# Unused buffers between the weights of a fused convolution and two-layer-pair kernel

## The reference, cut to what matters

```python
# x: (2, 4096, 192); weight: (8, 7); w_in: (192, 2048); w_out: (2048, 192), two sets of these
w = softmax(weight, axis=-1)                               # 8 heads, 7 taps
x_pad = concat([zeros(B, 6, D), x], axis=1)
x = sum over k of w[head, k] * x_pad[:, s + k, channels of head]   # causal convolution
# first pair of layers
h = x @ w_in
g = where(h >= 1, h, where(h <= -1, 0, (h + 1) ** 2 / 4))
x = g @ w_out
# second pair of layers
h = x @ moe2_w_in
g = h * sigmoid(1.702 * h)
out = g @ moe2_w_out                                       # (8192, 192)
```

## Time and profile before

| what | value |
|---|---|
| median of three runs | 1173.59 us (1173.38 to 1175.2) |
| the profiled execution | 1176.4 us, of which the span from first to last instruction is 1174.6 |
| mean granted TensorE clock | 0.999 of full speed |
| matmuls recorded | 9382 |
| moved by DMA | 31.27 MB |

### The profile page before, as it was taken

The page is one execution under the profiler, slowest core; times in us unless marked ns, Lnnn a source line. Parts: engine busy times, 40 slices in busy tenths (PEclk is TensorE's granted clock), DMA queues, the critical chain, the costliest instruction groups (busy, mean ns, idle before and its releaser), DMA issues.

```text
span 1174.6 us, 25920 instructions
## 1 busy us (share of the span) xinstructions
PE 1146.1 (98%) x9382; PEld 1011.3 (86%) x9382; DVE 844.6 (72%) x1206; ACT 799.3 (68%) x1510; POOL 432.3 (37%) x425
## 2 busy tenths in 40 slices
PE   7999999999999999999999999999999999999998
PEld 4767898998988889888888889889898888999987
DVE  6877768686776868768686786867768686676633
ACT  4866676767758677686766767677686766855554
POOL 5897626080440805327071350905317071000000
PEclk9999999999999999999999999999999999999999
DMA  6312101001010000101001010010101000000001
GB/s 193 97 37 75 35 1 48 1 10 40 1 48 1 15 35 2 47 1 48 2 8 41 1 49 1 12 37 1 49 1 48 1 7 9 2 15 2 14 2 28
DMA packets 63857, 31.27 MB, mean 27 GB/s; under 512 B 56084, under 2 KB 60562, under 8 KB 63760
## 3 DMA queue, kind: packets, MB, share of 16 engines
q1 hardware_dynamic: 63760, 29.80, 9.6%
HBM read 23.09 MB, written 6.29 MB: 25 GB/s over the span
## 4 chain that ended last, share of the span: by engine, by line
PE 73%; DVE 8%; ACT 8%; issue 5%; POOL 4%; SPq 1%; DMA 0%; DVEq 0%; ACTq 0%; POOLq 0%
PE acc_all L764 3%; PE acc_all L756 2%; PE acc_all L742 2%; PE acc_all L761 2%; PE acc_all L759 2%; PE acc_all L767 2%; DVE g_lo L1115 2%; PE h_all L697 2%; PE h_all L699 2%; PE h_all L694 2%; ACT clip L938 2%; PE h_all L701 2%; PE h_all L703 2%; PE acc_all L738 2%; PE acc_all L740 2%
## 5 line engine op out<-in xcount | busy, mean ns | idle before, releaser
L1115 DVE TENSOR_TENSOR g_lo<-gate,g_hi 128x512 fp32r<-128x512 f32 x232 | 205.1, 884 | 92.2 <-ACT g_hi L944 87.3
L1121 DVE TENSOR_TENSOR g_lo<-h_all,g_hi 128x512 fp32r<-128x512 f32 x256 | 175.7, 686 | 124.8 <-ACT h_all L955 122.5
L944 ACT ACTIVATE g_hi<-gate 128x512 fp32r<-128x512 f32 x232 | 146.5, 632 | 166.2 <-DVE gate L1109 131.4
L938 ACT ACTIVATE clip<-clip,half 128x512 f32<-128x512 f32 x256 | 184.9, 722 | 60.5 <-DVE clip L1100 58.0
L952 ACT ACTIVATE g_hi<-h_all 128x512 fp32r<-128x512 f32 x256 | 152.9, 597 | 94.6 <-PE h_all L705 66.7
L510 POOL TENSOR_TENSOR x_conv<-x_in,tap_w 128x384 f32<-128x384 f32 (+1 forms) x29 | 24.7, 872 | 515.9 <-ACT raw L990 513.4
L1100 DVE TENSOR_SCALAR clip<-h_all 128x512 f32<-128x512 f32 x256 | 174.9, 683 | 20.8 <-PE h_all L703 17.3
L517 POOL TENSOR_TENSOR x_conv<-x_conv,prod 128x384 f32<-128x384 f32 (+1 forms) x174 | 187.5, 1098 | 1.6
L1109 DVE TENSOR_TENSOR gate<-h_all,clip 128x512 f32<-128x512 f32 x232 | 160.5, 692 | 35.7 <-ACT clip L938 24.1
L510 POOL TENSOR_TENSOR prod<-x_in,tap_w 128x384 f32<-128x384 f32 (+1 forms) x174 | 176.4, 1038 | 4.2
L955 ACT ACTIVATE h_all<-h_all 128x512 f32<-128x512 f32 x256 | 151.6, 592 | 0.0
(11 more groups left out here) (281 smaller groups left out, 4763.2 us busy)
## 6 DMA issues: line engine op xcount, KB each, us to landing
x_in<-in_x SPq DMA_DIRECT2D x14, 960.0 KB, 4.7
out_y<-raw SPq DMA_DIRECT2D x360, 16.0 KB, 1.4
raw<-in_moe_w_out SPq DMA_DIRECT2D x6, 384.0 KB, 3.5
raw<-in_moe_w_in SPq DMA_DIRECT2D x4, 512.0 KB, 4.5
raw<-in_moe_w_in SPq DMA_DIRECT2D x8, 256.0 KB, 4.8
stage<-in_moe_w_out SPq DMA_DIRECT2D x2, 384.0 KB, 7.4
x_in<-in_x SPq DMA_DIRECT2D x1, 768.0 KB, 8.7
x_in<-in_x SPq DMA_DIRECT2D x2, 283.5 KB
```

Of the source, the lines that this page charges most:

```text
L938: nc.scalar.activation(c, c, ACT.Square, bias=half[:, :], scale=0.5).then_inc(square_ready, 1)
L944: nc.scalar.activation(g1_hi[step.s % G_RING][:, :], gate1_of(step)[:, :], ACT.Copy).then_inc(g1_hi_ready, 1)
L1115: nc.vector.tensor_tensor(g1_lo[k][:, :], gate1_of(step)[:, :], g1_hi[k][:, :].bitcast(FP32), ALU.subtract).then_inc(g1_lo_ready, 1)
L1121: nc.vector.tensor_tensor(g2_lo[k][:, :], bank2(step)[:, :], g2_hi[k][:, :].bitcast(FP32), ALU.subtract).then_inc(g2_lo_ready, 1)
```

## The change

Five buffers are added that no instruction reads or writes. `sb(name, [P, size // 4])` takes `size` bytes in each partition, so that all buffers after it begin that much later. Nothing else is changed. By the words of the change, the streamed operands begin at 0 of 512 bytes with it, in_hi and w_down too, in_lo at 32, rest_hi at 448 and rest_lo at 256.

```diff
+        def shift(name, size):
+            sb(name, [P, size // 4])
+
+        shift("to_in_hi", 384)
         in_hi = [sb(f"in_hi{m}", [P, FF], FP32R) for m in (1, 2)]
+        shift("to_in_lo", 32)
         in_lo = [sb(f"in_lo{m}", [P, FF], FP32R) for m in (1, 2)]
+        shift("to_rest_hi", 416)
         rest_hi = [sb(f"rest_hi{m}", [P, FF], FP32R) for m in (1, 2)]
+        shift("to_rest_lo", 320)
         rest_lo = [sb(f"rest_lo{m}", [P, FF], FP32R) for m in (1, 2)]
+        shift("to_w_down", 256)
         w_down = [sb(f"w_down{m}", [P, F_TILES, 2 * D], FP32R) for m in (1, 2)]
```

## The result

| | before | with the change |
|---|---|---|
| median | 1173.49 us (10 runs) | 1177.80 us (10 runs) |
| ratio | 1 | 1.0037, 95% interval 1.0027 to 1.0047 |
| profiled execution | 1176.4 us, span 1174.6 | 1177.45 us, span 1175.7 |
| shortest step (5th percentile of 231) | 4306 ns | 4333 ns |
| median step | 4333 ns | 4360 ns |

The kernel became 4.3 us slower (3.2 to 5.5 by the interval); faster was forecast. The profiled execution of before lay 2.9 us over its median, so the two spans show only 1.1 us of it. The steps are read from the starts of the first matmul of `end_up` (L694, now L703; all lines of PE are nine further down).

What follows compares the result with a forecast made beforehand. PE's matmul pace was taken to bound the kernel, with waits for g_lo in 28% of steps. From the profiled 1176.4 us, 6.0 came off, giving 1170.4, or 1167.5 against the runs' median; DVE, ACT and DMA at zero; range 1127 to 1183.

Steps and rivals of the forecast that it cites:

- the separation into absolute and relative movement: All operands leave 128 of 512 bytes; only in_lo, rest_hi and rest_lo move against the stream, 1256 of 4700 slots.
- C: Rival, up pairs: weight loads at 32, 448 and 256 meet the stream and one halts; 1181 us, at most 1186; chance 0.20.
- Price of a slot: Step pricing each PE matmul slot whose weights move against the stream: half of the 13.4 ns rest vanishes, -6.7 ns.
- the 13.4 ns over 512 columns: Part of each 227 ns PE matmul beyond 213.3 ns for its columns, 32 cycles; taken as changeable by addresses.
- the term of -8.4 us (6.0 arriving): PE's gain: 1256 slots at 6.7 ns, of which 0.72 reaches the kernel's time.
- B: Rival, every matmul: the 13.4 ns is a fixed price that knows no addresses, so nothing changes; 1173.6 us; chance 0.29.
- 1160 paired slots: Paired steps: in_lo twice, rest_hi twice, rest_lo once, 5 of 19 pairs over 232 steps; 96 single slots came on top.
- 0.72: Share of PE's gain taken to arrive, since 28% of the steps wait for g_lo at L742.
- Rival D: All 4700 slots: streams start at a 512-byte edge, so aligning removes the whole rest; 45 us, 1128.5 us; chance 0.13.

Runs made afterwards that it cites:

- e1: Kernel before plus one unused 384-byte buffer ahead of in_hi, so every weight and streamed operand begins at 0 of 512 bytes: ratio 1.0003.
- e2: The change without its first buffer: same distances between operands, all standing 384 bytes lower; ratio 1.0021 against the kernel before.
- e5: Kernel before with only rest_lo moved, 256 bytes from the place of the streamed operands: ratio 0.9994.
- m1: Separate kernel of matmuls alone, 40 per group, weights' and stream's starts varied in 32-byte steps: 226.7 ns at distances 0 and 256, up to 234.2 at others.
- m2: Separate kernel, PE alone, rings of ten weights, some moved, also narrower weights: ten matmuls 2266.7 ns with none moved, 2286.7 with one at 32.
- e8: Kernel before with only w_down moved, 32 bytes from the place of the streamed operands: ratio 1.0102, shortest step 4380 ns.
- e7: Kernel before with all five kinds of weights 32 bytes from the place of the streamed operands: ratio 1.0136, shortest step 4431 ns.
- e11: All weights 32 bytes away, in a kernel with the loop's convolution and ScalarE moves cut down: 1190.52 us against 1168.88 for that lighter kernel unshifted.

## Why the prediction was wrong

**What was right.** PE's pace is the term that moved; the medians on DVE and ACT stayed within 2 ns; the separation into absolute and relative movement, with the absolute one at nothing, holds (e1, e2). Of the three kinds that I took as moved against the stream, in_lo and rest_hi count and rest_lo does not (e5, 0.9994). The rival that came nearest, C, had the sign and the place, the up pairs, but not the 256 bytes of rest_lo, which are free; its price was 1181 us against 1177.8. Its picture, a load that meets the stream and halts one of them, is not shown: the runs show that the distance counts, not what halts.

**The step that failed is "Price of a slot".** I took the 13.4 ns over 512 columns as something that a distance could give back, and put half of it, -6.7 ns, on the moved slots. In these runs it is the floor for 512 columns of fp32r. m1 has no offset below 226.7 ns, bf16 shows that 10.9 of the 13.4 ns go away with the type and not with the place, and m2 that they don't go away with fewer columns of weights. The kernel before stood on the best distance, with all weights at 0. From a best place every move costs nothing or something: 20 ns for one moved weight by itself. So the term of -8.4 us (6.0 arriving) had the wrong sign: PE lost about 7 us, of which 4.3 arrived.

The trace of before could not show another distance, but it held one sign that can be read now: in the stretch of the earlier trace rows every start came 226 or 227 ns after the last. At bad distances m1's starts are uneven (231 and 235 in turns at 32, 227 to 241 at 128). And distance 0 for all weights is no typical place but a special one, best or worst; half the rest as a gain from leaving it had no row behind it. B and C deserved most of the chance.

**The slots.** I counted 1160 paired slots at one price each. In truth a moved weight that stands alone is paid for over some four matmuls, 20 ns in all, and 256 bytes are free. in_lo and rest_hi together cost 27 ns a step: 27 x 231 = 6.2 us, and about 1 us in the stretches with one stream (10 matmuls in 2306 ns against 2266 at the start, 2327 against 2293 in the tail).

**What arrives.** I said 0.72, from the share of steps without a wait. Measured: 4.3 of 7 us, 0.6, with the change; 11.6 of 17 us, 0.7, in e8; 16.0 of 31, 0.5, at 32 everywhere. The waits for g_lo shrink, and so does what the second half of down_both had lost before, as e7 and e11 show; in e11, with hardly any change in the waits, 21.6 of 31 arrive. My 0.72 let all arrive in the steps that don't wait and nothing in the others, and left the second half of down_both out; that 0.6 came near it is luck. I also took 231 intervals between the 231 rows of L742; there are 230, 4.434 us each, so the waits of before were 24 us and not 20. No sum hangs on it.

**Rival D** fell with e1: with everything aligned at 0 the shortest step is 4306 ns as before, so the rest stays. That 32 elements and 32 cycles agreed was chance. **The rule of the Trainium skill** that I set on B's side, "TensorE: Matmul & The Clock Gate", section "Step-by-step: what each phase is for" (a weight load takes no read bandwidth from the running matmul), would give every distance the same pace. It holds here for bf16 at the two distances that were run (0 and 32) and not for fp32r: 226.7 to 234.2 ns by nothing but the distance of the two. Its 216 ns for 512 columns is what bf16 showed, 215.8; for fp32r the measurement decides, 226.7.

**What stays open:** why 0, 144 and 256 bytes are free and the others not, what the 26 cycles are that fp32r has over bf16 (226.7 - 215.8 ns), why a disturbance lasts four matmuls, and why neighbouring ones cost less or more than their sum. Nor is it settled against which stream the distance counts, the one that runs while the weights load or the one that they are loaded for. One place in m1 speaks for the former: where weights and stream go together from 0 to 32, and then from 32 to 64, each matmul's own two operands have distance 0, and still the eight starts around the change come late by 32 and 33 ns in all. At distance 0 the tail (2293 ns for ten) and the second half of down_both are slower than 226.7 a matmul for a reason that no run shows. No placement tried beats the kernel before.

## What to carry to other kernels

Measure the floor before pricing a gain: if all matmuls already come at one even pace, that pace is more likely the best case than a hidden loss. With fp32r operands of 512 columns start weights and streamed operands at the same place within 256 bytes (buffer sizes that are multiples of 256 do it by themselves), and look at the distance between the starts of matmuls, not at their durations, which stayed at 0.38 to 0.40 us at every distance. Where a bound engine also waits at times, part of a slower pace is taken back elsewhere: here three to five tenths.

## What the runs showed of the hardware

- fp32r, 512 columns: 226.7 ns at the best distances, 233.2 at 32 bytes, 234.2 at 96 and 352; bf16 215.8 at 0 and at 32.
- 384 columns don't notice 32 bytes and notice 128 less: 173.4 ns at 0, 173.3 at 32, 176.1 at 128. With 256 columns the order turns: 119.7 at 0, 118.3 at 32.
- One weight at another distance costs 20 ns in all (48 cycles of 2.4 GHz), spread over some four matmuls. One at 32 with one at 448 behind it costs 41 in a ring of ten, and 27 for two such places in the kernel's order; two at 32 in a row cost 53.
- Two halves of the array side by side follow the same table as one stream alone, behind the first few pairs of a group: 226.7 ns at 0 and 256, 233 at 32, 229 at 448.
